# The hidden products of two dense layers by one level of Strassen's scheme, behind an attention kernel

## The reference

```python
def reference(q, k, v, moe_w_in, moe_w_out, moe2_w_in, moe2_w_out):
    scores = where(block_i >= block_j, q @ k.T / 8, -1e9)        # (4, 8, 576, 576)
    x = softmax(scores) @ v                                      # to (2304, 512)
    h = x @ moe_w_in                                             # (2304, 2048)
    x = (h * clip(h + 3, 0, 6) / 6) @ moe_w_out
    h = x @ moe2_w_in
    return (h * tanh(log1p(exp(h)))) @ moe2_w_out
```

## Time and profile before

| | |
|---|---|
| median of 3 runs | 1023.36 us (1022.04 to 1027.18) |
| the profiled execution, own time | 1022.14 us |
| its span | 1020.3 us |
| instructions in it | 16901, of which PE 5700 matmuls |
| busy: PE, DVE, ACT, POOL | 98%, 65%, 52%, 27% |
| granted clock of PE, mean | 0.997 |
| moved by DMA | 78.89 MB, mean 77 GB/s |

### The profile page before, as it was taken

One profiled execution on the slowest core, in us unless ns is written; L12 is line 12 of the kernel. 1 busy time (PEld: TensorE's weight loads), 2 busy tenths in 40 slices (PEclk: granted clock), 3 DMA queues, 4 the chain that ended last, 5 costly groups with the idle time before them and its releaser, 6 DMA issues.

```text
span 1020.3 us, 16901 instructions
## 1 busy us (share of the span) xinstructions
PE 995.0 (98%) x5700; PEld 931.1 (91%) x5700; DVE 662.3 (65%) x1280; ACT 530.9 (52%) x1161; POOL 279.7 (27%) x296
## 2 busy tenths in 40 slices
PE   6999999989999999999999999999999999999998
PEld 5888888889999999999999999999999999999996
DVE  5889889857332222222323559978888888888876
ACT  6889889846232222232323546555555465555553
POOL 7889889926022031130210200101001000010000
PEclk9999999989999999999999999999999999999999
DMA  6877886448121020120200342001000010000000
GB/s 156 238 184 212 212 208 169 101 142 257 39 73 52 20 81 23 54 69 0 88 28 31 132 140 75 24 1 48 16 31 23 8 39 23 0 31 0 32 1 31
DMA packets 42261, 78.89 MB, mean 77 GB/s; under 512 B 8032, under 2 KB 27616, under 8 KB 42208
## 3 DMA queue, kind: packets, MB, share of 16 engines
q1 hardware_dynamic: 36080, 68.48, 23.8%
q10 hardware_dynamic: 6128, 9.73, 2.6%
HBM read 59.24 MB, written 18.95 MB: 77 GB/s over the span
## 4 chain that ended last, share of the span: by engine, by line
PE 90%; DVE 4%; POOL 2%; issue 2%; ACT 1%; DMA 1%; SPq 0%; DVEq 0%; POOLq 0%
PE psum L525 38%; PE psum L500 13%; PE psum L502 13%; PE psum L501 13%; PE psum L451 4%; PE psum L430 4%; PE psum L406 3%; PE psum L411 3%; DMA qkin<-in_qk 0%; PE psum L409 0%; ACT prob L599 0%; POOL xraw L1002 0%; POOL xlo L1008 0%; DVE gsplit L845 0%; DVE wlo_early L832 0%
## 5 line engine op out<-in xcount | busy, mean ns | idle before, releaser
L1008 POOL TENSOR_TENSOR xlo<-xraw,xhi 128x384 f32 (+1 forms) x48 | 58.4, 1220 | 599.5 <-ACT xhi L659 599.5
L878 DVE SCALAR_TENSOR_TENSOR gbuf<-ebuf,psum 128x384 f32<-128x384 f32 x96 | 53.0, 552 | 218.3 <-ACT ebuf L711 218.3
L711 ACT ACTIVATE ebuf<-psum,three 128x384 f32<-128x384 f32 x96 | 55.7, 581 | 241.9 <-PE psum L502 241.9
L500 PE MATMUL psum<-xhi,whi_early 128*128 (+1 forms) x384 | 129.7, 338 | 1.3 <-POOL xlo L1008 1.3
L502 PE MATMUL psum<-xhi,wlo_early 128*128 (+1 forms) x384 | 129.4, 337 | 0.0
L501 PE MATMUL psum<-xlo,whi_early 128*128 (+1 forms) x384 | 129.2, 337 | 0.0
L502 PE MATMUL psum<-xhi,wlo_late 128*128 (+1 forms) x384 | 129.0, 336 | 0.0
L500 PE MATMUL psum<-xhi,whi_late 128*128 (+1 forms) x384 | 128.9, 336 | 0.0
L501 PE MATMUL psum<-xlo,whi_late 128*128 (+1 forms) x384 | 128.7, 335 | 0.0
L684 ACT ACTIVATE gsplit<-gbuf 128x384 fp32r<-128x384 f32 x192 | 100.1, 521 | 54.9 <-DVE gbuf L899 53.4
L845 DVE SCALAR_TENSOR_TENSOR gsplit<-gbuf,gsplit 128x384 fp32r<-128x384 f32 x192 | 123.0, 640 | 4.2 <-ACT gsplit L684 3.5
(11 more groups left out here) (89 smaller groups left out, 2298.2 us busy)
## 6 DMA issues: line engine op xcount, KB each, us to landing
wraw<-in_w SPq DMA_DIRECT2D x32, 512.0 KB, 3.5
qkin<-in_qk SPq DMA_DIRECT2D x43, 288.0 KB, 4.4
xraw<-attn_t SPq DMA_DIRECT2D x24, 384.0 KB, 3.3
attn_t<-late SPq DMA_DIRECT2D x44, 144.0 KB, 3.2
ystage<-in_qk SPq DMA_DIRECT2D x20, 288.0 KB, 4.5
xraw<-r_d SPq DMA_DIRECT2D x48, 96.0 KB, 3.3
x_t<-ystage ACTq DMA_DIRECT2D x24, 192.0 KB, 1.9
xraw<-x_t SPq DMA_DIRECT2D x24, 192.0 KB, 2.4
```

The source lines that it names most:

```text
L500: pe.matmul(bank(f % HB, TB), hi, x_part(xhi, blk, c), start=(c == 0), stop=False)
L711: nc.scalar.activation(ebuf[f % 2][:, :], bank(f % HB, TB), ACT.Relu, bias=three[:, 0:1]).then_inc(act_ready, 1)
L878: nc.vector.scalar_tensor_tensor(out=gbuf[f % 2][:, :], in0=e, scalar=6.0, in1=h, op0=ALU.min, op1=ALU.mult).then_inc(g_ready, 1)
L1008: nc.gpsimd.tensor_tensor(x_part(xlo, blk, c), xraw[c][:, 0, :], x_part(xhi, blk, c).bitcast(F32), ALU.subtract).then_inc(x_lo, 1)
```

## The change

h is made for a pair of feature tiles (256 features) at a time, and for a block of 384 tokens. The operands are halved: features (a pair), width (2 x 256) and tokens (2 x 192). Winograd's form of Strassen's scheme gives the four quadrants of h from seven products instead of eight. Each product is 2 width chunks x 3 passes over 192 columns.

- POOL forms four mixes of the weights (S1 to S4, 256 columns each, `mix_w`) and four of x (T1 to T4, 384 columns each, `mix_x`). The seven operands of each side are then split into high and low: 2816 columns of weights for a pair (with w_out), 2688 columns of x for a block, against 2048 and 1536 before.
- Of the seven products, pairs share a PSUM bank. ACT copies the first product and the state of two banks to SBUF (`snap_products`), and the first quadrant; DVE adds U and two quadrants (`sum_u`, `sum_quads`), POOL the fourth (`sum_last_quad`). h then lies in SBUF (`hbuf`).
- The elementwise work goes over 768 columns at once, with h from SBUF. In layer 1 the low part of g is POOL's, as is that of x; in layer 0 both are DVE's.
- The weights of a layer no longer fit whole, so each layer goes over its 6 blocks twice, with 4 pairs (half the features) each time: 24 passes of a block, 96 steps of a pair. The first pass's y goes to memory and is added in the second; x goes to memory and is loaded again.
- SP now issues the stores of y too.
- In attention, the weights of pair 0 (with its mix) are split at heads 3 and 6, those of pair 1 at head 9; x of block 0 is mixed on POOL at heads 29 and 30, and its low parts are DVE's.

```diff
-            for c in range(DC):
-                hi, lo = (w_part(t, f, c * P, P) for t in (whi, wlo))
-                pe.matmul(bank(f % HB, TB), hi, x_part(xhi, blk, c), start=(c == 0), stop=False)
-                pe.matmul(bank(f % HB, TB), hi, x_part(xlo, blk, c), start=False, stop=False)
-                last = pe.matmul(bank(f % HB, TB), lo, x_part(xhi, blk, c), start=False, stop=(c == DC - 1))
...
+PRODUCTS = ((A11, B11, BANK_X, True), (S2, T2, BANK_Y, True), (S1, T1, BANK_Z, True), (S3, T3, BANK_V, True),
+            (A12, B21, BANK_X, False), (S4, B22, BANK_Z, False), (A22, T4, BANK_V, False))
...
+            def h_products(g):
+                blk, p = g // PAIRS, g % PAIRS
+                pair = g // PASS * PAIRS + p
+                for k, (a, b, pb, first) in enumerate(PRODUCTS):
+                    if k == M1 and g % PASS < PAIRS:
+                        pe.wait_ge(w_lo, 3 * pair + 2)
+                    if p == 0 and k in (M1, M6, M7):
+                        pe.wait_ge(x_lo, 4 * blk + {M1: 1, M6: 3, M7: 4}[k])
+                    if k == M1 and g > 0:
+                        pe.wait_ge(snapped, SNAP * g)
+                    elif k in (M6, M5, M7) and g > 0:
+                        pe.wait_ge(quad_ready, QUAD * (g - 1) + k)
+                    elif k in (M2, M3, M4):
+                        pe.wait_ge(snapped, SNAP * g + k - M7)
+                    for c in range(2):
+                        hi, lo = (t[p][:, (2 * a + c) * P:(2 * a + c + 1) * P] for t in (whi, wlo))
+                        xh, xl = (x_quad(t[blk % 2], b, c) for t in (xhi, xlo))
+                        pe.matmul(bank(pb, HT), hi, xh, start=(first and c == 0), stop=False, skip_group_check=True)
+                        pe.matmul(bank(pb, HT), hi, xl, start=False, stop=False, skip_group_check=True)
+                        last = pe.matmul(bank(pb, HT), lo, xh, start=False, stop=(c == 1), skip_group_check=True)
+                    last.then_inc(product, 1)
...
+            for s in range(NPAIR):
+                for g in h_steps(s):
+                    h_products(g)
...
+                y_matmuls(s)
...
+                if n == 3:
+                    split_w_hi(0, 0)
+                    split_w_hi(0, 1)
...
+                if i == 1:
+                    act.wait_ge(w_mixed, 4 * (pair + 1))
...
+            for s in range(-1, NPAIR):
+                second = s + 1 if s >= SWITCH + 1 and s + 1 < NPAIR else None
+                if second is not None:
+                    exp_minus_ln(second)
...
+                for g in h_steps(s):
+                    snap_products(g)
+                    if layer_of(g) == 0:
+                        relu_h(g)
+                    else:
+                        exp_h(g)
+                split_w_out_hi(s)
+                if second is not None:
+                    split_g_hi(second)
...
+                split_w_in_hi(s)
+                for g in h_steps(s):
+                    split_next_x_hi(g)
+                    if layer_of(g) == 1:
+                        ln_n(g)
...
+            def sum_u(g):
...
+                nc.vector.tensor_tensor(usum[:, :], snaps[:, 0, :], bank(BANK_Y, HT), ALU.add).then_inc(quad_ready, 1)
...
+                nc.vector.scalar_tensor_tensor(out=gbuf[:, :], in0=tbuf[:, :], scalar=-1.0, in1=hbuf[g % 2][:, :],
+                                               op0=ALU.mult, op1=ALU.mult).then_inc(g_ready, 1)
...
+                if second is not None:
+                    times_r(second)
...
+                for g in h_steps(s):
+                    sum_u(g)
+                if second is not None:
+                    n_times_r(second)
+                for g in h_steps(s):
+                    sum_quads(g)
+                    if layer_of(g) == 0:
+                        relu6_times_h(g)
+                split_w_out_lo(s)
+                if second is not None:
+                    mish_times_h(second)
+                elif s < SWITCH:
+                    split_g_lo(s + 1)
+                split_w_in_lo(s)
+                for g in h_steps(s):
+                    if layer_of(g) == 0:
+                        split_next_x_lo(g)
+                    else:
+                        cap_and_n(g)
...
+            def split_g_lo(g):
+                pool.wait_ge(g_hi, g + 1)
+                nc.gpsimd.tensor_tensor(glo[g % 2][:, :], gbuf[:, :], ghi[g % 2][:, :].bitcast(F32), ALU.subtract
+                                        ).then_inc(g_lo, 1)
...
+                if w_in_at(s) is not None:
+                    mix_w(w_in_at(s))
+                for g in h_steps(s):
+                    sum_last_quad(g)
+                    prepare_next_x(g)
+                if second is not None:
+                    split_g_lo(second)
```

More of the change, by code:

```diff
@@ new lines, in x_mix, with w_group, w_source, w_in_at @@
+        def x_mix(i):
+            return xraw[:, i, 1, :].rearrange("p (k t) -> p k t", k=2)
+        W_GROUPS = ((0, 3 * A_COLS), (3 * A_COLS, 4 * A_COLS), (W_IN, W_OUT))
+        def w_group(t, i):
+            c0, n = W_GROUPS[i]
+            return t[:, c0:c0 + n]
+        def w_source(pair, i):
+            if i == 1:
+                return wmix[:, :]
+            return wraw[(2 * pair + i // 2) % WS][:, 0:W_GROUPS[i][1]]
+        def w_in_at(s):
+            late = {-1: 2, 1: 3}
+            if s in late:
+                return late[s]
+            k = s + PAIRS
+            return k // PASS * PAIRS + k % PASS if k >= PASS and k // PASS < 4 and k % PASS < PAIRS else None
@@ L203, in build, with w_out_at @@
+        def w_out_at(s):
+            late = {-1: 1, 0: 2, 2: 3}
+            if s in late:
+                return late[s]
+            return w_in_at(s - 1) if s > PAIRS else None
         Y_COLS = (TB, D)
@@ new lines, in split_w_hi, with split_x_hi @@
+                nc.scalar.activation(w_group(whi[p], i), w_source(pair, i), ACT.Copy).then_inc(w_hi, 1)
+            def split_x_hi(blk, i):
+                if i < 2 and blk < NB:
+                    act.wait_ge(x_scaled, DC * (blk + 1))
+                elif i < 2:
+                    act.wait_ge(x_block_loaded, 16 * (blk - NB + 1))
+                else:
+                    act.wait_ge(x_mixed, 4 * blk + (2 if i == 2 else 4))
+                if blk >= 2:
+                    act.wait_ge(product, PROD * PAIRS * (blk - 1))
+                elif blk == 1:
+                    act.wait_ge(av_done, AV * NHEAD)
+                    for s in range(OS):
+                        act.wait_ge(o_stored[s], stored(s, NHEAD))
+                nc.scalar.activation(x_group(xhi[blk % 2], i), x_source(i), ACT.Copy).then_inc(x_hi, 1)
```

848 lines of the change are left out of this document (475 added, 373 removed).

## The result

The changed kernel takes **1270.97 us** (median of 4 runs, 1267.13 to 1271.69) against 1022.71 for the kernel before beside it: a ratio of 1.241 [1.236, 1.245], so slower by 24%. The profiled run took 1271.43 us, its span is 1269.6.

The account below looks back on a forecast made before the run. PE was taken to bound the dense layers, with turns between POOL and DVE setting layer 1's step after the change. 1022.1 + 44 + 114 + 20 + 5 + 6 + 14 + 7 + 3 + 3 = 1238 us; range 1095 to 1285.

Parts of the forecast that it names:

- The products, +44: PE, both dense layers: 4032 matmuls at 0.110 us replace 2304 at 0.1732 us for h, +44 us.
- Rival (c): PE's products: columns, not weight loads, set the pitch (0.080 us), making the kernel faster at 979 us; chance 0.03.
- The layer-1 step, 11.2 us: Layer 1: POOL and DVE taking strict turns stretch a step from PE's 8.83 to 11.2 us, +114 us.
- rival (a): Layer 1: turns are rarer or fall in free time, PE sets the pace, terms 114 and 20 vanish: 1104 us; chance 0.18.
- rival (b): Layer 1: PE's clock falls after its idle time in each step, 86 us more, 1324 us; chance 0.08.
- The first pairs, +3: Start of the dense layers: a product waits behind DVE's reciprocal, y of pair 0 behind pair 1's weights, +3 us.
- The change of layers, +5: Where layer 0 gives way to layer 1: a further cost beside the weight-split steps, +5 us.
- The weight steps, +20: Four layer-1 steps splitting the second pass's weights: DVE and POOL work holds the way, ACT adds 3 us; +20 us.
- the shared way: SBUF access where POOL and two-SBUF-input DVE operations take turns; 9.7 us held per layer-1 step against PE's 8.8.
- Attention, +21: Attention: ACT's weight splits wait twice some 7 us for POOL's mix, +14; x ready later at the end, +7.
- Layer 0, "nothing" plus 6: Layer 0: shared turns cost nothing; last x splits about 1 us late in five blocks, with change of pass, +6.
- The tail, +3: End of the kernel: one DVE sum more in a row, +3 us.

Follow-up runs that it names:

- the run with 4 columns: The changed kernel with POOL's layer-1 mixes and low parts of x cut to 4 columns of each group: 1198.87 us, ratio 1.168.
- the best version: Changed kernel; later: attention's second weight mix, x block 1, layer-1 pass-change weight splits, mixes behind h's quadrant; x lows on DVE; block 13 loaded first: 1193.58 us.
- the first experiment: The changed kernel with ACT and DVE splitting attention's mixed weights at heads 5 and 11 instead of 3 and 9: 1254.72 us, ratio 1.223.

## Why the prediction was right, and where it was off

The direction and the mechanism were right; 1238 was 33 us too low, and errors of both signs stand behind it: the steady steps of layer 1 were put 22 us too high and all other stretches together 55 too low, so that the sum came as near as it did is in part luck.

- **The products, +44.** Right, and 4 short. 42 matmuls at 0.111 us instead of 0.110, and 0.04 us a step more around the matmuls of y, so 0.54 us a step in layer 0 (8.86 against 8.32) and 0.455 in layer 1 (8.83 against 8.375): 48 x 0.995 = +48. Rival (c), the columns as the pitch, is out by the run with 96 columns. The change has 7/8 of the multiplications but 7/4 as many matmuls, and here a matmul of 192 columns isn't half of one of 384 (0.173 us) but two thirds.
- **The layer-1 step, 11.2 us.** The mechanism is shown by the run with 4 columns, in which what rival (a) describes is left: 8.87 us a step. The size was high: the 40 steps without weights took 10.68. The walk of "strict turns" gave 2.4 us of idle a step; measured are 1.2 of standing and 0.66 of slower matmuls. The long step is the term that was over-sized: I walked the four steps of a block as if nearly each had a full list; the steps of a usual block are 9.4, 10.3, 10.1 and 14.5 us, three short ones and a long one, and after block 22, with no next x to prepare, the last run at 8.83.
- **PE's clock, rival (b).** It did not replace the forecast but came with it: 26.3 us in the 40 steps where (b) had 86 for layer 1, and by the same split 10.5 in the weight steps, 14.5 in the first pairs and 7.8 at the change of layers, some 60 of the 249 us in all (what was slow before in the first pairs, at most 4, is in it). By the granted clock alone, half of PE's working time at 0.50, it is 22.0, 10.5, 12.2 and 7.3, some 52. The earlier trace rows showed slower matmuls behind a wait of 2.55 us, so the forecast should have carried a term for each such wait it foresaw; as a rival it could only be all or nothing.
- **The first pairs, +3: the step that failed most,** measured 25 us above the terms. It priced DVE and ACT at pair 0, and said of the loads that each lands in 2 to 4 us "with a block of 35 us around it, 0". Block 1 has no block around it: its loads are issued as attention ends. POOL, given both x's additions and h's last quadrant, stood for a DMA with h behind it. That is shown for 6.0 us; the rest is, by the traces and not by an experiment, two more waits for weights (3.30 us behind ACT's high parts, 3.9 for DVE's low parts) and the clock, for none of which the prediction had a term.
- **The change of layers, +5,** measured 14 us above the terms. The same step of the argument failed: SP's queue was counted as free, and there the load of x stood behind weight loads that wait for buffers. 7.1 us are shown to be that load, and 4.5 in the best version the weight mix ahead of h's quadrant; the rest stays open.
- **The weight steps, +20,** right in size (66.9 us against 64.8 for four), but by luck. The reason given, that both engines hold the shared way, is not the main one: DVE's operations in these steps are stretched by 7.6 us in all over their times alone (0.96, 1.22 and 0.56 us), and the steps take 31.6 over PE's pace. The order of ACT's and DVE's work accounts for 8.5 of these, the mix ahead of the quadrant for 4.1 more, and by the granted clock 10.5 are slower matmuls, which overlaps with both; the rest stays open.
- **Attention, +21,** measured +24, with 7 us of spread between profiled runs; its part of 14 is shown by the first experiment (14.3 at h(0)). The 7 at its end were not tried apart.
- **Layer 0, "nothing" plus 6:** the 41 steps are 9 us over; 3 of these are the pitch (0.54 us a step for 0.46). The other 6 lie beyond the 6 that were priced: 11.9 over PE's own in all, 8.4 of it in the three steps y(21) to y(24) of the change of pass, where PE stands 4.10 us for DVE's last split of x.
- **The tail, +3,** measured +4.4 with the moved h taken off: right.

## What to carry to other kernels

Count matmuls and their weight loads, not multiplications: a scheme that halves the columns of a matmul must also halve the loads, and with 0.11 us for a matmul whether it has 96 columns or 192, Strassen's 7/8 of the work cost 12% more here on the engine it was meant to relieve, before any wait. Its additions then went to the two engines that take turns, inside the chain between a product and its use.

Where an engine gets a duty that belongs to the chain (a quadrant of h, a snapshot) beside one that waits for a DMA (the next x, the next weights), put the chain's duty first and look where the DMA is late, in the first block and at each change of stage. There this forecast was 39 us too low, while it was 22 too high for the steady steps of layer 1; moving such duties or their load gave back 6.0, 7.1 and, in the best version, 11.5 us. And a wait long enough to drop the clock costs more than its length: in layer 1 some half again (26.3 us on 47.6).

## What was not expected of the hardware

- With matmuls of 96 columns, PE recorded busy without a gap (100.00 of 100 us), it was granted 0.85 of the clock in that window of layer 0, and 0.80 over layer 1; with 192 columns in the same window 1.00. Less work per load made the kernel 83 us slower.
- DVE's cap (one tensor input, 768 columns of SBUF) is stretched by POOL like the operations with two inputs: 0.56 us to 2.20, 1.17 on the mean. The prediction counted it as part of a chain and not among the five that hold the way. The Trainium skill ("GPSIMD Engine Reference", section "1. Specifications") says that DVE and GpSimd contend in a 2-port mode or with two SBUF inputs; that the cap runs in such a mode would fit, and no run here shows it.
- The start of h(0) varied by 7 us between profiled runs with the same attention.
